# A three-stage token mixer on one core: GpSimd takes low parts, softmax steps and wrap copies, and the last slot joins its window

## The reference

```python
# 1: a per-token softmax over 7 taps for each of 8 heads, then a causal weighted sum of 7 tokens
w = exp(weight_gen - max); w = w / (sum(w) + 1e-09)
x = einsum('bshk,bskhg->bshg', w, x_unf)
# 2: token shift and a gated squared-ReLU network, 192 -> 1024 -> 192
xk = mu_k * x + (1 - mu_k) * x_prev
xr = mu_r * x + (1 - mu_r) * x_prev
x = sigmoid(xr @ w_r) * (relu(xk @ w_k) ** 2 @ w_v)
# 3: 192 -> 1024, a depthwise convolution of 3 taps along the sequence, a gate, 1024 -> 192
h = relu(x @ w_in)
conv_out = sum over k of conv_w[k] * h shifted by k - 1   # zeros at both ends of a batch
out = (h * sigmoid(conv_out)) @ w_out
```

## Time and profile before

| | us |
|---|---|
| median of 3 runs | 737.31 (736.87 to 737.6) |
| profiled execution | 737.71 |
| its span on the core | 735.9 |
| PE busy | 696.3 (95%) |
| DVE busy | 681.4 (93%) |
| ACT busy | 648.5 (88%) |
| POOL busy | 3.6 |

### The profile page before, as it was taken

The page is one execution under the profiler, slowest core; times in us unless marked ns, Lnnn a source line. Parts: engine busy times, 40 slices in busy tenths (PEclk is TensorE's granted clock), DMA queues, the critical chain, the costliest instruction groups (busy, mean ns, idle before and its releaser), DMA issues.

```text
span 735.9 us, 10798 instructions
## 1 busy us (share of the span) xinstructions
PE 696.3 (95%) x3531; PEld 590.7 (80%) x3531; DVE 681.4 (93%) x1057; ACT 648.5 (88%) x1351; POOL 3.6 (0%) x9
## 2 busy tenths in 40 slices
PE   0788999999999999999999999999999999999995
PEld 0677988888888888888888887888888888888984
DVE  7999999999999999998999999999999999786776
ACT  3788999899989989898989889898998989897985
POOL 1000000000000000000000000000000000000000
PEclk9999999999999999999999999999999999999999
DMA  6701101010102001010101101010200101000000
GB/s 157 231 16 40 55 12 54 16 55 22 54 1 71 5 22 55 22 53 23 55 1 28 48 23 53 23 54 0 76 1 23 54 22 44 22 1 1 22 23 21
DMA packets 9053, 28.76 MB, mean 39 GB/s; under 512 B 1038, under 2 KB 4136, under 8 KB 8870
## 3 DMA queue, kind: packets, MB, share of 16 engines
q1 hardware_dynamic: 8840, 28.05, 11.6%
q10 hardware_dynamic: 158, 0.03, 0.0%
HBM read 21.69 MB, written 6.39 MB: 38 GB/s over the span
## 4 chain that ended last, share of the span: by engine, by line
PE 75%; DVE 18%; issue 4%; ACT 1%; DMA 1%; SPq 0%; DVEq 0%; ACTq 0%
PE up L320 32%; PE od L436 20%; PE dn L384 4%; PE dn L400 4%; PE dn L407 4%; PE dn L404 4%; PE dn L403 4%; DVE att L830 3%; PE dn L406 3%; DVE prod L818 3%; DVE cv L927 3%; DVE cv L937 2%; PE mid L291 1%; DVE kq_lo L894 1%; DVE gat L946 1%
## 5 line engine op out<-in xcount | busy, mean ns | idle before, releaser
L436 PE MATMUL od<-wo_sb,gat 128*128 128x192 f32 x1040 | 188.9, 329 | 6.4 <-DVE gat L946 6.3
L436 PEld LDWEIGHTS od<-wo_sb,gat 128*128 128x128 f32 x1040 | 173.8, 191 | 17.7 <-DVE gat L946 5.4
L927 DVE SCALAR_TENSOR_TENSOR cv<-h,prm,cv 128x512 f32<-128x512 f32 (+2 forms) x144 | 98.4, 693 | 19.9 <-ACT cv L606 19.7
L894 DVE TENSOR_TENSOR kq_lo<-ksq,kq_hi 128x512 fp32r<-128x512 f32 (+2 forms) x144 | 89.3, 632 | 14.3 <-ACT kq_hi L572 13.8
L937 DVE SCALAR_TENSOR_TENSOR cv<-h,prm,cv 128x512 f32<-128x512 f32 (+2 forms) x144 | 98.3, 693 | 0.4
L606 ACT ACTIVATE cv<-h,prm 128x512 f32<-128x512 f32 (+2 forms) x144 | 97.0, 675 | 0.0
L818 DVE TENSOR_TENSOR prod<-xin,wgt 128x768 f32<-128x768 f32 (+2 forms) x108 | 95.6, 886 | 1.0
L830 DVE TENSOR_TENSOR att<-att,prod 128x768 f32<-128x768 f32 (+2 forms) x108 | 95.4, 883 | 0.0
L946 DVE TENSOR_TENSOR gat<-h,cv 128x512 f32<-128x512 f32 (+2 forms) x144 | 90.6, 631 | 0.4 <-ACT cv L613 0.2
L597 ACT ACTIVATE h<-up 128x512 f32<-128x512 f32 (+2 forms) x144 | 79.9, 556 | 11.3 <-PE up L320 10.0
L613 ACT ACTIVATE cv<-cv 128x512 f32<-128x512 f32 (+2 forms) x144 | 83.7, 584 | 6.0 <-DVE cv L937 5.3
(11 more groups left out here) (111 smaller groups left out, 1351.6 us busy)
## 6 DMA issues: line engine op xcount, KB each, us to landing
...
```

The lines of the kernel that those rows point to most:

```text
L436: mm = nc.tensor.matmul(o, lhs, wo_sb[:, c, :], start=(c == 0 and b % 2 == 0), stop=(c == NC - 1), skip_group_check=(b % 2 == 1))
L894: nc.vector.tensor_tensor(ring(kq_lo, c, n), ring(ksq, c, n), ring(kq_hi, c, n).bitcast(F32), ALU.subtract).then_inc(kql_ok, 1)
L927: nc.vector.scalar_tensor_tensor(o, win(w, c, -1), prm[:, 3 + c:4 + c], o, ALU.mult, ALU.add)\
```

## The change

Four things change together.

1. **w_in's low parts on POOL.** DVE's four subtractions of 128x512 become two of 128x1024 on POOL. The semaphore `wi_split` is what `up2` of group 0 then waits for.
2. **Softmax parts 1 to 4.** The subtraction and the product go to POOL; maximum, sum, add and reciprocal stay on DVE. The front half is written a step earlier than the back half, and the DMA of part 1's weights is issued ahead of w_in instead of behind it. Part 0 stays whole on DVE.
3. **The end.** The last slot is convolved in window 17, which grows from 2 to 3 slots (its next slot is a wrap copy at column AFTER); window 18 is slot 0 alone (the slot before it is a wrap copy at AHEAD). POOL makes the copies in halves of 4 chunks, and `carry` of window 17 is dropped.
4. **The order.** All three lists are written anew and the loops run over other numbers; an index such as i - 12 only shifts them. Each call keeps its distance in groups to the others of its engine, except `softmax_front`.

```diff
@@ window geometry
+        def win_slots(w):
+            return 1 if eq(w, NG) else size(w) + (1 if eq(w, NG - 1) else 0)
+        ALONE = KEEP + P
+        HALF = NC // 2
+        AFTER = (SIZES[-1] + 2) * P
+        AHEAD = 0
         def win(w, c, off):
+            at = P + off * P
             if eq(w, NG):
-                return last_pair(c, off)
-            return h3[:, c, (1 + off) * P:(1 + off) * P + win_cols(w)]
+                at = AHEAD if off < 0 else ALONE + off * P
+            return h3[:, c, at:at + win_cols(w)]
@@ SP
+            load_weights(SM_ENDS[1], SM_ENDS[2], wg2_in)
             load_up_weights(sp, w_in, 2, wi_in)
             sp.wait_ge(wi_in, 48)
...
+            load_weights(SM_ENDS[2], TPP + 1, wg3_in)
@@ gpsimd
+            def split_wi(n):
+                rows = (P, P)[n]
+                pool.wait_ge(w_cast, 3 + n)
+                nc.gpsimd.tensor_tensor((wi_lo, wi2_lo)[n][0:rows, :], raw_w(2 + n, 0, rows),
+                                        (wi_hi, wi2_hi)[n][0:rows, :].bitcast(F32), ALU.subtract).then_inc(wi_split, 1)
+            def softmax_differences(n):
...
+                pool.wait_ge(sm_max, n)
+                nc.gpsimd.tensor_tensor(wgt_rows(lo, hi), wgt_rows(lo, hi), vals(hi - lo)[1], ALU.subtract)\
+                    .then_inc(sm_sub, 1)
+            def softmax_quotients(n):
...
+                pool.wait_ge(sm_exp, n + 1)
+                pool.wait_ge(sm_rec, n)
+                nc.gpsimd.tensor_tensor(wgt_rows(lo, hi), wgt_rows(lo, hi), vals(hi - lo)[1], ALU.mult).then_inc(sm_ok, 1)
...
+            pool.wait_ge(h_keep, NC)
+            for n in range(2):
+                half = slice(n * HALF, (n + 1) * HALF)
+                pool.wait_ge(h_free, NC * n_windows(NG - 1) - (HALF if n == 0 else 0))
+                nc.gpsimd.memset(h3[:, half, AFTER + PPB - 1:AFTER + P:PPB], 0.0).then_inc(wrap_fix, 1)
+                nc.gpsimd.tensor_copy(part_of(half, AFTER, 0), part_of(half, ALONE, 1)).then_inc(h_wrap, 1)
+            for n in range(2):
+                half = slice(n * HALF, (n + 1) * HALF)
+                pool.wait_ge(h_ok, NC * (NG - 1) + (n + 1) * HALF)
+                pool.wait_ge(tap, NC * n_windows(NG - 1) + (n + 1) * HALF)
+                nc.gpsimd.memset(h3[:, half, AHEAD:AHEAD + P:PPB], 0.0).then_inc(wrap_fix, 1)
+                nc.gpsimd.tensor_copy(part_of(half, AHEAD, 1), part_of(half, AFTER - P, 0)).then_inc(h_last, 1)
@@ tensor: the list (also shown in rows below)
-                down1(i - 1, 7)
-                down2(i - 2, 5)
...
+                up2(i - 13, 6)
+                down2(i - 14, 7)
+                up2(i - 13, 7)
+                up1(i - 12, 0)
+                r_part(i - 12, 1)
...
@@ scalar
-                if not window(w):
+                if not window(w) or eq(w, NG - 1):
                     return
...
-            act.wait_ge(wrap_fix, 2)
+            act.wait_ge(h_keep, NC)
@@ vector
+                if eq(w, NG):
+                    dve.wait_ge(h_last, c // HALF + 1)
+                    dve.wait_ge(wrap_fix, c // HALF + 3)
...
+                if n >= 1:
+                    nc.vector.reduce_max(v, wgt_rows(lo, hi), axis=AX_X).then_inc(sm_max, 1)
+                    return
...
+                if n >= 1:
+                    nc.vector.reciprocal(v, v).then_inc(sm_rec, 1)
+                    return
...
-            nc.vector.tensor_copy(h3[:, :, 2 * P:3 * P - 1], h3[:, :, KEEP + P + 1:KEEP + 2 * P]).then_inc(h_wrap, 1)
-            nc.vector.tensor_copy(h3[:, :, KEEP + 1:KEEP + P], h3[:, :, P:2 * P - 1]).then_inc(h_wrap, 1)
```

More of the change, by code:

```diff
@@ L427, in down2 @@
                     pe.wait_ge(wo_in, 16)
-                if c == 0 and not eq(w, 1):
+                if c == 0 and not eq(w, 1) and not eq(w, NG):
                     pe.wait_ge(o_ok, 2 * n_windows(w))
@@ L479, in _ @@
+                down1(i - 12, 5)
+                t_part(i - 11, 2)
+                down2(i - 13, 3)
+                down1(i - 12, 6)
+                down1(i - 12, 7)
+                down2(i - 13, 4)
+                add_small(i - 12)
+                down2(i - 13, 5)
+                down2(i - 13, 6)
             pe.wait_ge(id_ok, 2)
@@ L763, in step @@
-                k_square(i, 4)
-                if i == -2:
-                    cast_wr()
-                double(i + 1)
-                k_cast(i, 4)
-                gate_sigmoid(i - 1, 4)
-            for i in range(-2, NG + 2):
+                h_relu(i - 12, 1)
+                carry(i - 13, 7)
+                h_relu(i - 12, 2)
+                first_tap(i - 12, 1)
+                h_relu(i - 12, 3)
+                xr_hi_part(i - 11, 2)
+                h_relu(i - 12, 4)
+                first_tap(i - 12, 2)
@@ L771, in _ @@
+                first_tap(i - 11, 0)
+            for i in range(8, NG + 14):
                 step(i)
-            act.wait_ge(wrap_fix, 2)
+            act.wait_ge(h_keep, NC)
             for c in range(NC):
```

405 lines of the change are left out of this document (196 added, 209 removed).

## The result

| kernel | median (lowest to highest), us | ratio to before, 95% interval |
|---|---|---|
| before | 737.32 (736.87 to 737.60) | |
| after | 745.02 (744.47 to 745.77) | 1.0104 [1.0088, 1.012] |

The change makes the kernel 7.7 us **slower**. The forecast was 734.3 us, 3 us faster; the result lies outside the range. The profiled execution has a span of 743.6 us, 7.7 more than before.

What follows compares the result with a forecast made beforehand. PE was taken to bound the middle, DVE the start and the end. End -3.8, start +1.7 and middle -0.9 summed to -3.0 us, from the median 737.3 to 734.3 us; range 726.5 to 739.5, the forecast's own 731.5 to 737.

Steps and rivals of the forecast that it cites:

- the end: Windows 17 and 18: fewer columns, no gap between windows, earlier start, fewer last products; -3.8 us, bounds -2.5 and -4.8.
- new order, start: Group 0's step: DVE following its new list waits for `k_cast` and the end of `down1`, some 1 us more.
- new order, rest: Plain groups: the chain to `up2` fits with some 0.4 us to spare and no handoff is late; 0 us.
- arithmetic on POOL, start and middle: Start: 4.3 us leave DVE, POOL holds it +5.0 us; middle: softmax stalls change by -0.9 us.
- the walk: Window 18 on DVE, counted from instruction starts: 0.86 us per chunk, 6.9 us for eight.
- the end gains nothing: Rival: wrap copies come late and window 18 waits for POOL as it did for DVE; 737.5 us, chance 0.06.
- What POOL does to DVE: Start: POOL's two-input work takes 7.0 us and holds DVE, save some 2 us of waiting anyway; +5.0 us.
- The forecast's case: DVE's instructions with two SBUF tiles stand still beside POOL's reads at two passes an element; 734.3 us, chance 0.42.
- Nobody disturbed: Rival: POOL does not hold DVE, so -3.8 - 3.3 - 2.8 = -9.9; 727.4 us, chance 0.28.
- Three passes: Rival: POOL's reads at three passes an element hold DVE 8.4 us at the start; 741.6 us, chance 0.12.
- The middle: Groups with softmax parts 2 to 4, which stall PE 2.8 us; -0.9 us, bounds -2.8 and +3.
- Boundary too tight: Rival: y's low parts come 0.3 us late in each of 14 full groups; 738.5 us, chance 0.12.

Runs made afterwards that it cites:

- b_tail: Kernel before, own order, with the change's new end and window 17's output copies on ACT behind window 18's first four taps: 735.60 us.
- a_dve_taps: Changed kernel with POOL's arithmetic back on DVE (wrap copies stay) and window 17's output copies behind window 18's first four taps: 738.69 us.
- h_start: a_dve_taps, but TensorE, ScalarE and VectorE follow the old order up to `up2` of group 3, the new order from there: 735.16 us.
- a_taps_first: Changed kernel with ACT's copy of window 17's outputs moved behind the first four first_tap of window 18: 741.69 us.
- a_all_dve: Changed kernel with w_in's low parts and the softmax subtractions and products back on DVE; POOL keeps the wrap copies: 741.53 us.
- p_sub: Kernel before plus four idle POOL subtractions of 128x1024 on a scratch tile in the start: 742.93 us.
- b_wi_pool: Kernel before with only w_in's subtractions moved, two of 128x1024 on POOL for four of 128x512 on DVE: 739.15 us.
- b_best: b_tail with maxima and differences of softmax parts 2, 3 and 4 a step earlier on DVE, part 1 and loads unmoved: 734.40 us.

## Why the prediction was wrong, step by step

| step | predicted, us | measured, us | from |
|---|---|---|---|
| the end | -3.8 | +1.4 | b_tail less before (-1.9), plus the copies ahead of the taps (+3.3); between the traces of before and after +1.1 |
| new order, start | +1.0 | +3.5 | a_dve_taps less h_start; 0.4 to 1.2 with the clock up throughout |
| new order, rest | 0 | -0.4 | h_start less b_tail |
| arithmetic on POOL, start and middle | -0.2 (-4.3 + 5.0 - 0.9) | +3.0 to +3.5 | a_taps_first less a_dve_taps; after less a_all_dve |
| sum | -3.0 | +7.5 to +8.0 | the change: +7.7 |

**The end** is the largest miss, 5.2 us. The step that failed is "`first_tap` of window 18 needs only kept data". True of its data; but I did not look at what stands ahead of it on ACT. `o_copy` of window 17 does, and what that waits for comes from DVE's last gate of window 17. It stood there before the change too, and waited:

```profile
720.52 0.49 ACT L622 ACTIVATE o_sb<-od 128x384 f32<-128x384 f32 x1 [1.24 <-PE od L436]
```

The first tap of window 18 followed it at 720.90, and the 0.72 us that DVE waits for that tap in the earlier trace rows are this wait; DVE's two copies and two clearings hid the rest. I counted the whole 2.67 us between the windows as gone. With DVE's copies away the wait of ACT's copy stands free, and it costs 3.3 us. I had seen the like for the window before ("ACT copied the outputs of window 16 ahead of the first taps") and did not ask it again here. The rest is size. With the queue mended it is 26.6 us from `up2` to the end (710.36 to 737.0 in a_dve_taps), where I had 25.0: the first convolution came 2.0 us behind `up2`, not 1.5, and three convolution steps beside a wrap copy took 1.0 us instead of 0.6. I had priced those copies as something to wait for and not as something that holds DVE, though I had taken that very rule for the subtractions. Window 18, at 7.16 us, was within 0.3 of the walk. The rival "the end gains nothing" had the number nearly right and the cause wrong: POOL's last wrap copy is done at 728.1 us, 4 us before window 18 starts. (As a sum, an end worth 0 in place of -3.8 gives 734.3 + 3.8 = 738.1 us, where I wrote 737.5.)

**What POOL does to DVE** was right in kind. The forecast's case was that DVE's instructions stand still beside POOL's, and they do. The size was not: DVE is held 6.6 us at the start, where the term had 7.0 less 2.0 = 5.0. The full 7.0 would have been close. The 2 us that I took off, as time in which DVE would have waited anyway, were 0.7: `up2` of group 3 comes 1.6 us later than with the arithmetic on DVE (a_all_dve), so with the 4.3 us that left DVE 5.9 of the 6.6 were paid. POOL itself reads for longer, 6.20 + 1.47 + 1.36 = 9.0 us: the two softmax steps take the 1.4 us of two passes, but w_in's subtractions 3.1 us each where I took 2.1. p_sub shows that a subtraction free of DVE takes 1.9 to 2.4 us and that POOL too is made to wait; DVE is held 2.2 us for each of the long ones, so I take the rest of the 3.1 to be POOL's own wait. The other part of the 3.5 us, 1.9, is in the middle. "Nobody disturbed" is refuted by p_sub and b_wi_pool. "Three passes" had the 3.1 us, but a hold of 8.4 us, and gave 741.6 us since it had the end at -3.8.

**The middle** was to gain 0.9 and lost: the stalls went from 2.8 to 3.5 us. I had written that if POOL holds DVE "the last two parts stall again, by about as much as now", which is 0, and took -0.9, a mean with the case in which POOL disturbs nobody, though the forecast's own case was the hold. POOL's steps there take 1.6 to 3.0 us each, not 1.4 to 2.1. With the arithmetic on DVE the stalls are 1.6 (a_all_dve). b_best shows that the idea was sound, that of the front half a step early, when nothing moves to POOL and part 1 stays: 1.2 us less than b_tail.

**The new order at the start** I walked with the old trace's durations and found 1 us. Such a walk keeps PE's clock where it was. It fell: 1.8 us of the 3.5 came back when PE was kept busy through the wait, and with the clock up throughout only 0.4 to 1.2 are left, about the 1 us of the walk. So what failed here is a term that the forecast did not have at all, the fall of the clock behind PE's new waits.

**Plain groups:** 41.70 for 41.67 us. "Boundary too tight" is refuted for them, and "0 us" was right. At 4 of the 14 full groups, beside softmax parts, the low part did come 0.3 us late.

**The chances.** Slower had 0.18, from rivals of one mechanism each. What came is three losses at once. The end came out beyond its bounds (-2.5 at worst), and the order at the start, for which I had given none, at three times its size.
